# Moving a capacity comparison behind a weight split at the seam of two expert layers, and sharing a copy

## The chip, the cores and the metric

The kernel runs on one core of one Trainium2 chip. The metric is the time of one execution on the device in microseconds, from the core's own clock. A core has five engines that run their own instruction streams and meet through semaphores: TensorE (PE in the profile) for matrix products, VectorE (DVE), ScalarE (ACT), GpSimd (POOL) and SyncE (SP). DMAs are issued from the queues of SyncE, ScalarE and GpSimd. Before the change the kernel takes 393.19 us (median of three runs, 393.05 to 393.44).

## The reference

Three stages, each feeding the next, on N = 1536 tokens (2 batches of 768) with 512 features:

```
attention   state = gamma[h] * state + k_t v_t^T ;  y_t = scale * q_t state      (8 heads of 64)
layer 0     tokens with x @ w_skip > 0 choose the expert argmax(x @ w_gate) of 8
            out = x + gate * (relu(x @ w1[e]) @ w2[e])      w1 512x1024, w2 1024x512; other tokens pass
layer 1     every token chooses e = argmax(x @ w_gate) of 8
            the first `capacity` tokens of each expert, in token order, are kept
            out = gate * (relu(x @ w1[e]) @ w2[e]) for the kept ones, 0 for the others
```

The capacity in layer 1 is what the changed comparison is about: a token is kept only if fewer than `capacity` tokens ahead of it chose the same expert. Capacity is an input (384 here). The result is float32.

## The kernel before

**Stages.** The attention runs in chunks of 128 tokens and is over at about 75 us. Layer 0 follows, to about 195 us, then layer 1 to the end. In both layers experts are processed one after the other (a "job"): the rows of an expert's tokens are gathered by an indirect DMA of GpSimd into `xg`, turned on TensorE into `ps_t` (features on the partitions), copied to SBUF, multiplied by w1 in groups of 512 columns into `ps_h` (two banks by turns), passed through relu and multiplied by w2 into `ps_y`. The rows go back by an indirect store. A layer is a loop over "windows" of 128 (layer 0) or 256 (layer 1) tokens of each expert; one window does for the inputs here. Layer 0 takes 128 rows of each expert at a time, layer 1 takes 256.

**Precision.** Layer 1 (and the w2 products of layer 0) splits each fp32 operand in two parts that TensorE can take in its faster format: a high part (`w_hi`, `x_hi`, `h_hi`), which is a cast by ScalarE, and the rest (`w_lo`, `x_lo`, `h_lo`), which VectorE computes as original minus high part. A product is then three matmuls: w_hi x_hi, w_lo x_hi, w_hi x_lo. A job's weights come in four chunks of 1 MB (`raw`, loaded by SyncE, two jobs deep): 0 and 1 are w1, 2 and 3 are w2. Each has a split of 128x2048 elements on ScalarE (L732) and on VectorE (L1044). The matmuls of w1 are on L1425, those of w2 on L1453 and L1469. TensorE may start a chunk's matmuls when `hi_done` and `lo_done` of the chunk have come, and may write a bank of `ps_h` again when `h_hi` and `h_lo` of the group two before are made.

**Layer 1's choices while layer 0 ends.** The logits of layer 1 need the rows that layer 0 puts out. Those of the last two experts of layer 0 (the "late" rows, LATE = 2) come last, so their choices are made apart (`choose_late`, `rank_late`). The order of the tokens then has to be known over both kinds: `cross_counts` counts, with 24 small matmuls of the mask `above` with the late rows' choices `hot1`, how many late tokens stand ahead of each token and chose the same expert. `find_fits` (three small VectorE steps, L1149 to L1151) compares the sum of both counts with the capacity and writes `fits`. ScalarE stores `fits` to `flags` in HBM (L810), GpSimd gathers from it (L611), and VectorE uses it in layer 1's second job (L1125). `map_next` (L1342) is another set of small matmuls, which finds for each slot of an expert the token that goes there; its result in `ps_e` becomes the row numbers `slot_in` (L1167, L1169), with which GpSimd gathers the second job's rows (L539). The first job's rows are gathered earlier, by `gather_first` (L580). They come from `x_rows` as it stands then; the rows of the last expert of layer 0 that belong to them are added by matmuls of `late_hot` (L1566) into `ps_t`, on which `turn_first` (L1391) then accumulates the others.

**The order at the seam.** Each engine's queue is written out by hand, and it is strictly in order:

- TensorE, end of layer 0: L1566, then `above_ready`, `cross_counts` (which signals `crossed`), then `slots_ready` and the late map (signals `slots_mapped`). Layer 1: wait for `first_in` (the gather), `turn_first` (signals `first_half` after half of it and `turned` at its end), two filler matmuls on a zero tile (`keep_clock`, L1240), then `hidden(first, 0)`: it waits for `x_hi_done`, `hi_done[0]`, `lo_done[0]`. Its first 8 matmuls are w_hi x_hi, the next 8 w_lo x_hi, and before the third 8 it waits for `x_lo_done`.
- VectorE, end of layer 0: `choose_late(1)`, `rank_late(1)`, `late_hot`, `place` (L920), then a wait for `crossed` and `find_fits`. Layer 1: `split(first, 0)`, a wait for `slots_mapped`, L1167 and L1169, `split_x`, `split(first, 1)`, `relu` (h_lo, L1055) of group 0, `split(first, 2)`, and so on.
- ScalarE: the casts of chunks 0 and 1 of the first job, then `copy_first`, which copies both halves of `x_hi` (L745), the cast of chunk 2, h_hi of group 0 (L750), a wait for `fits_ready`, the store of the flags, the exponential, the cast of chunk 3.
- GpSimd: `gather_first` (L580, two DMAs), the stores of the last job of layer 0 (L564, L572), waits for stores and gathers to land, then in layer 1 the wait for the ids and the gathers of the second job.
- SyncE: the loads of the second job's weights wait for `first_in`.

`Chain` is a helper that lets each of a row of dependent VectorE steps signal a semaphore and wait for it; it counts its steps, and that count per window stands in the code (47 and 18). `hold` is a wait that also counts up a semaphore nobody reads.

## Time and profile before

| | us |
|---|---|
| median of the runs | 393.19 |
| the profiled execution | 393.83 |
| its span, first to last instruction | 392.0 |
| TensorE busy | 380.6 |
| VectorE busy | 260.8 |
| ScalarE busy | 171.6 |
| GpSimd busy | 83.8 |

The table's first line is of executions without the profiler, the others of the one execution that was profiled. The span lies inside the execution's time. "Busy" counts the time in which an engine works on an instruction; matmuls overlap in the pipeline, so TensorE's busy time is not time at its peak. The granted TensorE clock was full (1.00) over the span. The chain of work that ended last is followed back from the last instruction, at each step to what released it; what lies on it sets the end.

### The profile page before, as it was taken

What the parts mean: (1) busy time and instruction counts of PE and PEld (TensorE: products, weight loads), DVE (VectorE), ACT (ScalarE), POOL (GpSimd) and SP (SyncE); (2) the same over time, 40 slices, a digit from 0 to 9 for tenths busy, and PEclk for the clock granted to TensorE, in tenths of its full rate; (3) what the DMA queues carried; (4) which work ended last, traced back from release to release, by engine and by line L of the source; (5) the groups of instructions that cost most, each with busy time, mean ns of one, the idle gap of its engine ahead of it and who ended that gap; (6) DMA issues with size and microseconds to landing.
All of it is one profiled execution on the core that took longest, in us unless ns stands there. A gap on an engine that the chain in (4) does not pass through costs nothing.

```text
span 392.0 us, 7630 instructions
## 1 busy us (share of the span) xinstructions
PE 380.6 (97%) x2853; PEld 341.2 (87%) x2853; DVE 260.8 (67%) x468; ACT 171.6 (44%) x218; POOL 83.8 (21%) x83
## 2 busy tenths in 40 slices
PE   8999999999999999999889999999999999999996
PEld 5888887788899889988679898989989899898983
DVE  2876877759998889879396847364474636547340
ACT  2454453515324532451464256455454644445410
POOL 5110000240454142331432021402204030030103
PEclk9999999999999999999999999999999999999999
DMA  7999998389999999809599988666748557440102
GB/s 244 367 380 383 348 350 288 73 317 399 390 387 390 390 386 360 299 7 361 165 346 354 352 306 253 228 225 205 246 179 287 183 207 247 152 163 2 53 0 89
DMA packets 56018, 101.55 MB, mean 259 GB/s; under 512 B 6693, under 2 KB 18469, under 8 KB 55856
## 3 DMA queue, kind: packets, MB, share of 16 engines
q1 hardware_dynamic: 46048, 85.67, 61.7%
q0 software_dynamic: 4576, 11.71, 8.8%
q10 hardware_dynamic: 5360, 3.70, 3.1%
q8 instruction: 23, 0.38, 0.4%
q14 instruction: 11, 0.09, 0.1%
HBM read 89.91 MB, written 12.73 MB: 262 GB/s over the span
## 4 chain that ended last, share of the span: by engine, by line
PE 93%; DVE 2%; DMA 2%; issue 1%; ACT 1%; SPq 1%; POOL 0%; DVEq 0%; ACTq 0%; POOLq 0%
PE ps_h L1425 38%; PE ps_y L1453 31%; PE ps_r L1300 3%; PE ps_s L1253 3%; PE ps_o L1288 3%; PE ps_u L1267 3%; PE ps_y L1469 3%; PE ps_t L1383 2%; PE ps_o L1280 2%; DMA k_in<-in_k_rows 2%; PE ps_h L1240 1%; DVE w_lo L1044 1%; PE ps_t L1566 1%; PE ps_t L1492 1%; PE ps_e L1342 0%
## 5 line engine op out<-in xcount | busy, mean ns | idle before, releaser
L1044 DVE TENSOR_TENSOR w_lo<-raw,w_hi 128x2048 fp32r<-128x2048 f32 x48 | 109.1, 2288 | 19.8 <-ACT w_hi L732 18.2
L732 ACT CAST w_hi<-raw 128x2048 fp32r<-128x2048 f32 x48 | 90.7, 1909 | 4.0 <-PE ps_y L1453 2.9
L1055 DVE SCALAR_TENSOR_TENSOR h_lo<-ps_h,h_hi 128x512 fp32r<-128x512 f32 x48 | 33.1, 690 | 63.1 <-ACT h_hi L750 53.1
L750 ACT ACTIVATE h_hi<-ps_h 128x512 fp32r<-128x512 f32 x48 | 28.8, 599 | 96.9 <-PE ps_h L1425 93.9
L1453 PE MATMUL ps_y<-w_hi,h_hi 128*128 128x512 f32 x176 | 70.7, 402 | 0.0
L1453 PE MATMUL ps_y<-w_hi,h_lo 128*128 128x512 f32 x176 | 68.8, 391 | 0.0
L1453 PE MATMUL ps_y<-w_lo,h_hi 128*128 128x512 f32 x176 | 68.7, 390 | 0.0
L1425 PEld LDWEIGHTS ps_h<-x_f,raw 128*128 128x128 f32 x512 | 58.5, 192 | 1.3 <-issue 0.7
L1425 PE MATMUL ps_h<-x_f,raw 128*128 128x128 f32 x512 | 58.9, 275 | 0.3 <-issue 0.3
L1425 PE MATMUL ps_h<-x_hi,w_hi 128*128 128x256 f32 x256 | 41.1, 283 | 1.6 <-DVE w_lo L1044 1.6
L1425 PE MATMUL ps_h<-x_hi,w_lo 128*128 128x256 f32 x256 | 41.0, 283 | 0.0
L1425 PE MATMUL ps_h<-x_lo,w_hi 128*128 128x256 f32 x256 | 41.0, 283 | 0.0
L539 POOL DMA_INDIRECT xg<-x_rows,slot_in x14 | 15.3, 1096 | 114.4 <-ACT yo L761 106.6
L1453 PEld LDWEIGHTS ps_y<-w_hi,h_lo 128*128 128x128 f32 x176 | 33.0, 188 | 7.2
L1453 PEld LDWEIGHTS ps_y<-w_lo,h_hi 128*128 128x128 f32 x176 | 33.2, 188 | 5.9
L1453 PEld LDWEIGHTS ps_y<-w_hi,h_hi 128*128 128x128 f32 x176 | 33.1, 188 | 5.9
L1425 PEld LDWEIGHTS ps_h<-x_hi,w_hi 128*128 128x128 f32 x256 | 35.6, 191 | 2.5 <-issue 1.9
L1425 PEld LDWEIGHTS ps_h<-x_lo,w_hi 128*128 128x128 f32 x256 | 35.3, 192 | 0.0
L1425 PEld LDWEIGHTS ps_h<-x_hi,w_lo 128*128 128x128 f32 x256 | 35.2, 192 | 0.0
L539 POOL DMA_INDIRECT xg<-x_rows,slot_id x8 | 15.3, 1907 | 70.6 <-issue 47.5
L1077 DVE SCALAR_TENSOR_TENSOR product<-yo,w_wide 128x512 f32<-128x512 f32 x48 | 30.3, 689 | 0.0
L564 POOL DMA_INDIRECT out<-yo,slot_out x16 | 16.1, 1003 | 39.0 <-ACT yo L761 20.9
(175 smaller groups left out, 429.7 us busy)
## 6 DMA issues: line engine op xcount, KB each, us to landing
raw<-in_moe_w SPq DMA_DIRECT2D x64, 1024.0 KB
q_t<-in_q_cols SPq DMA_DIRECT2D x16, 192.0 KB, 6.1
k_t<-in_k_cols SPq DMA_DIRECT2D x16, 192.0 KB, 6.0
x_rows<-rows ACTq DMA_DIRECT2D x8, 384.0 KB, 5.4
k_in<-in_k_rows SPq DMA_DIRECT2D x15, 192.0 KB, 6.5
v_in<-in_v_rows SPq DMA_DIRECT2D x15, 192.0 KB, 6.4
out<-zero SPq DMA_DIRECT2D x1, 2816.0 KB
w_wide<-w_next SPq DMA_DIRECT2D x1, 2048.0 KB, 14.3
```

The lines of the kernel that those rows point to most:

```text
L539: nc.gpsimd.indirect_dma_start(out=job.rows_of(t), out_offset=None, in_=x, in_offset=bass.IndirectOffsetOnAxis(ap=ids[t], axis=0), bounds_ ...
L564: nc.gpsimd.indirect_dma_start(out=target, out_offset=bass.IndirectOffsetOnAxis(ap=rows_at, axis=0), in_=yo[:, job.par, t * DM:(t + 1) * D ...
L732: nc.scalar.copy(w_hi[c], raw[:, 4 * job.par + c, :]).then_inc(hi_done[c], 1)
L750: nc.scalar.activation(h_hi[:, g * 512:(g + 1) * 512], ps_h[:, g % 2, :], ACT.Relu).then_inc(h_hi_done[i], 1)
L1044: nc.vector.tensor_tensor(w_lo[c], raw[:, 4 * job.par + c, :], w_hi[c].bitcast(F32), ALU.subtract).then_inc(lo_done[c], 1)
L1055: nc.vector.scalar_tensor_tensor(out=h_lo[:, cols], in0=ps_h[:, g % 2, :], scalar=0.0, in1=h_hi[:, cols].bitcast(F32), op0=ALU.max, op1=AL ...
L1077: last = nc.vector.scalar_tensor_tensor(out=product[:, e], in0=yo[:, job.par, 0:DM], scalar=1.0, in1=w_wide[:, e], op0=ALU.mult, op1=ALU.m ...
L1253: last = pe.matmul(ps_s[:, p, a, c * P:(c + 1) * P], k_t[part, hp, toks], q_t[part, hp, toks], start=True, stop=True)
L1267: last = pe.matmul(ps_u[:, c * P:(c + 1) * P], k_dec[:, p, c].rearrange("p a d -> p (a d)"), v_in[:, hp, half * HC + c].rearrange("p a d - ...
L1288: last = pe.matmul(ps_o[a * D:(a + 1) * D, c * P:(c + 1) * P], v_in[:, hp, c0 + c, a, :], probs[:, p, a, c, :], start=False, stop=True, sk ...
L1425: last = pe.matmul(dst, wt[:, kk * QF + fb * P:kk * QF + (fb + 1) * P], xt[:, kk, :], start=(kk == 0 and z == 0 and not (first and g == 0 ...
L1453: last = pe.matmul(ps_y[:, t, :], ht, wt, start=(fb == 0 and z == 0), stop=(fb == 2 * QB - 1 and z == 2))
```

## The change

It does four things. The three steps of `find_fits` move in VectorE's queue from the end of layer 0 to layer 1's first job, behind `split_x` and ahead of `split(first, 1)`. The counts of `cross_counts` go to columns 128 to 223 of the bank `ps_e`, where the maps are at columns 0 to 31, instead of a bank of `ps_y`; TensorE does the late map ahead of them, and one semaphore, `slots_mapped`, tells of both (`crossed` goes). ScalarE copies only the first half of the first `x_hi`; VectorE copies the second in a new step `copy_half`, on whose semaphore `x_half_done` it waits itself before `split_x`. TensorE waits for `x_half_done` beside `x_hi_done`. ScalarE's wait for `fits_ready` becomes a plain one on this window's count.

```diff
--- before.py
+++ after.py
@@ -37,6 +37,7 @@
 LATE = 2
 GL = G + LATE
 PRE = 2 * P
+CROSS = P
 
 
 class Layer:
@@ -281,7 +282,7 @@
         first_in = sem("first_in")
         first_half = sem("first_half")
         late_placed = sem("late_placed")
-        crossed = sem("crossed")
+        x_half_done = sem("x_half_done")
         fits_ready = sem("fits_ready")
         flags_stored = sem("flags_stored")
         flags_in = sem("flags_in")
@@ -737,13 +738,8 @@
                     nc.scalar.copy(dst, ps_t[:, 0:KD * cap].rearrange("p (k n) -> p k n", k=KD)).then_inc(x_hi_done[i], 1)
 
                 def copy_first(job):
-                    for h in range(2):
-                        if h == 0:
-                            act.wait_ge(first_half, w + 1)
-                        else:
-                            act.wait_ge(turned[1], job.n + 1)
-                        last = nc.scalar.copy(x_hi[:, 2 * h:2 * h + 2], ps_t[:, h * 2 * cap:(h + 1) * 2 * cap].rearrange("p (k n) -> p k n", k=2))
-                    last.then_inc(x_hi_done[1], 1)
+                    act.wait_ge(first_half, w + 1)
+                    nc.scalar.copy(x_hi[:, 0:2], ps_t[:, 0:2 * cap].rearrange("p (k n) -> p k n", k=2)).then_inc(x_hi_done[1], 1)
 
                 def relu(job, g):
                     wait_hidden(act, layer, job, g)
@@ -806,7 +802,7 @@
                         copy_first(first)
                         split(first, 2)
                         relu(first, 0)
-                        hold(act, fits_ready, first_fits)
+                        act.wait_ge(fits_ready, w + 1)
                         act.dma_start(flags.rearrange("(p g) e -> p g e", g=G), fits[:, 0:G]).then_inc(flags_stored, 16)
                         nc.scalar.activation(ex[:], below[:], ACT.Exp).then_inc(exp_done[1], 1)
                         split(first, 3)
@@ -829,7 +825,6 @@
                         scale_y(last_two[1], by_block=True)
                 n_win = win.count()
                 base = n_win * (E // 2)
-                first_fits = n_win
 
 
         @block.vector
@@ -1048,6 +1043,11 @@
                     dve.wait_ge(x_hi_done[1], job.n + 1)
                     nc.vector.tensor_tensor(x_lo[:], ps_t[:, 0:KD * cap].rearrange("p (k n) -> p k n", k=KD),
                                             x_hi[:].bitcast(F32), ALU.subtract).then_inc(x_lo_done[1], 1)
+
+                def copy_half(job):
+                    dve.wait_ge(turned[1], job.n + 1)
+                    nc.vector.tensor_copy(x_hi[:, 2:4], ps_t[:, 2 * cap:4 * cap].rearrange("p (k n) -> p k n", k=2)).then_inc(x_half_done, 1)
+                    dve.wait_ge(x_half_done, w + 1)
 
                 def relu(job, g):
                     dve.wait_ge(h_hi_done[i], job.n * layer.groups + g + 1)
@@ -1145,14 +1145,14 @@
                     nc.vector.tensor_tensor(first_id[:], first_found[:], found[:, :, 1, 0], ALU.add).then_inc(first_ids, 1)
 
                 def find_fits(chain):
-                    counts = [at.rearrange("p (g e) -> p g e", e=E) for at in (ps_g[:, PRE:PRE + G * E], ps_y[:, 1, 0:G * E])]
+                    counts = [at.rearrange("p (g e) -> p g e", e=E) for at in (ps_g[:, PRE:PRE + G * E], ps_e[:, CROSS:CROSS + G * E])]
                     chain.step(nc.vector.tensor_scalar(tmp[:, 0:G], counts[0], cap_f[:, 0:1], None, ALU.subtract))
                     chain.step(nc.vector.tensor_tensor(tmp[:, 0:G], tmp[:, 0:G], counts[1], ALU.add))
                     nc.vector.tensor_scalar(fits[:, 0:G], tmp[:, 0:G], 0.0, None, ALU.is_lt).then_inc(fits_ready, 1)
 
                 win = Windows(dve, layer)
                 with dve.Fori(0, win.reg) as w:
-                    wchain = Chain(dve, win_link[i], w, (47, 18)[i])
+                    wchain = Chain(dve, win_link[i], w, (45, 20)[i])
                     hold(dve, window_stored[i], w + 1)
                     first = Job(layer, base, w, 0, 0)
                     if i == 1:
@@ -1191,7 +1191,9 @@
                             last = nc.vector.tensor_tensor(above[:, j], repeat(iota_b[:, 0:P], 1, G), repeat(offset[:, j], 2, P), ALU.is_gt)
                         last.then_inc(above_ready, 1)
                     else:
+                        copy_half(first)
                         split_x(first)
+                        find_fits(wchain)
                         split(first, 1)
                         relu(first, 0)
                         split(first, 2)
@@ -1219,8 +1221,6 @@
                         nc.vector.tensor_scalar(late_hot[:], iota_b[:], rank1[:, G + 1:G + 2], late_first[:, 0:1], ALU.is_equal, ALU.mult
                                                 ).then_inc(late_placed, 1)
                         place(1, [G + 1]).then_inc(slots_ready[1], 1)
-                        dve.wait_ge(crossed, w + 1)
-                        find_fits(wchain)
                     else:
                         wchain.step(nc.vector.tensor_scalar(rank1[:], rank1[:], -float(cap), None, ALU.add))
                         place(1, range(GL)).then_inc(slots_ready[1], 1)
@@ -1331,9 +1331,9 @@
 
                 for g in range(G):
                     for j in range(LATE):
-                        last = pe.matmul(ps_y[:, 1, g * E:(g + 1) * E], above[:, j, g, :], hot1[:, G + j, :],
+                        last = pe.matmul(ps_e[:, CROSS + g * E:CROSS + (g + 1) * E], above[:, j, g, :], hot1[:, G + j, :],
                                          start=g + j == 0, stop=j == LATE - 1, skip_group_check=True)
-                last.then_inc(crossed, 1)
+                return last
 
             def map_next(groups):
 
@@ -1398,6 +1398,8 @@
 
                     if c == 0 and part[0] == 0:
                         pe.wait_ge(x_hi_done[i], job.n + 1)
+                        if first:
+                            pe.wait_ge(x_half_done, w + 1)
                     if i == 0:
                         pe.wait_ge(raw_landed[4 * job.par + c], job.all_half * 16 + 16)
                     else:
@@ -1565,10 +1567,10 @@
                         for kk in range(KD):
                             pe.matmul(ps_t[:, kk * 2 * P:(kk + 1) * 2 * P], yo[:, 1, kk * P:(kk + 1) * P], late_hot[:],
                                       start=kk % 2 == 0, stop=False, skip_group_check=True)
+                        pe.wait_ge(slots_ready[1], w * 3 + 3)
+                        map_next([G + 1])
                         pe.wait_ge(above_ready, w + 1)
-                        cross_counts()
-                        pe.wait_ge(slots_ready[1], w * 3 + 3)
-                        map_next([G + 1]).then_inc(slots_mapped[1], 1)
+                        cross_counts().then_inc(slots_mapped[1], 1)
                     else:
                         output_by_block(last_two[1])
                         for kk in range(0, KD, 2):
```

## Rows read from the trace of the kernel before

**Rows 1.** The page: TensorE's busy time, share, instructions; shares of the chain by engine.

```profile
PE 380.6 (97%) x2853; PEld 341.2 (87%) x2853; DVE 260.8 (67%) x468; ACT 171.6 (44%) x218; POOL 83.8 (21%) x83
...
PE 93%; DVE 2%; DMA 2%; issue 1%; ACT 1%; SPq 1%; POOL 0%; DVEq 0%; ACTq 0%; POOLq 0%
```

**Rows 2.** The chain that ended last, around the seam: start us, us, what.

```profile
193.82 1.32 PE ps_y L1334 x24
...
195.16 0.33 DVE tmp L1149
...
195.51 0.27 DVE tmp L1150
...
195.80 0.05 DVE fits L1151
...
196.43 2.30 DVE w_lo L1044
198.73 0.14 issue
198.87 11.75 PE ps_h L1425 x96
```

**Rows 3.** Timeline of the seam: start, us, engine, line, operation, [idle before <-releaser].

```profile
189.26 3.70 ACT L732 CAST w_hi<-raw 128x2048 fp32r<-128x2048 f32 x2 [0.26 <-issue]
...
190.58 1.02 POOL L580 DMA_INDIRECT xg<-x_rows,first_id  x1 [0.30 <-issue]
...
191.69 0.28 DVE L920 TENSOR_SCALAR slots<-iota_b,rank 128x256 bf16<-128x256 bf16 x1
...
193.23 1.00 POOL L572 DMA_INDIRECT next_rows<-next_lg,slot_row  x1 [0.30 <-issue]
...
195.38 1.06 PE L1391 MATMUL ps_t<-iw,xg 128*128 128x128 f32 x8 [0.93 <-DMA xg<-x_rows,first_id]
195.40 2.19 SPq L439 DMA_DIRECT2D raw<-in_moe_w  x4
...
196.04 1.08 ACT L745 CAST x_hi<-ps_t 128x512 fp32r<-128x512 f32 x2 [3.08 <-PE ps_t L1391]
...
196.28 1.03 PE L1240 MATMUL ps_h<-zero 128*128 128x256 f32 x4
196.43 2.29 DVE L1044 TENSOR_TENSOR w_lo<-raw,w_hi 128x2048 fp32r<-128x2048 f32 x1 [0.42 <-issue]
...
198.64 0.17 DVE L1167 TENSOR_SCALAR found_id<-ps_e 128x16 f32<-128x16 f32 x1
...
198.93 1.22 DVE L1049 TENSOR_TENSOR x_lo<-ps_t,x_hi 128x1024 fp32r<-128x1024 f32 x1
...
199.89 1.04 POOL L539 DMA_INDIRECT xg<-x_rows,slot_in  x1 [5.66 <-DVE slot_in L1169]
...
200.06 2.28 DVE L1044 TENSOR_TENSOR w_lo<-raw,w_hi 128x2048 fp32r<-128x2048 f32 x1
...
200.86 1.12 PE L1425 MATMUL ps_h<-x_lo,w_hi 128*128 128x256 f32 x8
201.24 2.00 POOL L539 DMA_INDIRECT xg<-x_rows,slot_in  x1 [0.31 <-issue]
...
202.02 0.60 ACT L750 ACTIVATE h_hi<-ps_h 128x512 fp32r<-128x512 f32 x1 [3.10 <-PE ps_h L1425]
...
202.65 0.69 DVE L1055 SCALAR_TENSOR_TENSOR h_lo<-ps_h,h_hi 128x512 fp32r<-128x512 f32 x1 [0.30 <-ACT h_hi L750]
```

**Rows 4.** Busy us of each engine in two stretches behind the seam, clock, DMA.

```profile
199.00:212.00 13.00, 13.00 (x103) 12.74 (x104) 10.62 (x13) 4.62 (x7) 5.05 (x4) 1.00 1.01 369
212.00:386.00 174.00, 174.00 (x1162) 158.39 (x1161) 96.81 (x95) 83.77 (x78) 29.39 (x29) 1.00 0.58 196
```

**Rows 5.** The waits from 198 to 216: who waited for whom, us, times, longest.

```profile
POOL fits L611 <- DMA flags<-fits: 5.0, 1, 5.0
```

## The prediction

> **What bounds the kernel now.** I read the page first: TensorE is busy 97% of the span and holds 93% of the chain that ended last [rows 1]. So time can only come from a spot where the chain leaves TensorE. The chain in order of time [rows 2] shows such a spot at the seam of the two layers. TensorE ends its last small matmuls of layer 0 at 195.14. Then the chain runs on VectorE: three steps of the capacity comparison from 195.16, the loop's change of layer, and the split of the first weight chunk (w_lo) from 196.43 to 198.73. TensorE begins layer 1's first expert at 198.87. From there the chain is TensorE alone, and the windows say the same: busy 13.00 of 13.00 us and 174.00 of 174.00 up to 386 [rows 4]. What TensorE starts earlier at 198.87 the end gets back in full, unless a new gap opens behind it.
>
> The timeline of the seam [rows 3] tells what else stood ready at 198.87. The first expert's rows are turned from 195.38 (TensorE had waited for their gather, the last wait before it) to 196.44. ScalarE copied them to x_hi until 197.12. The weight's high part was cast long before: two chunks from 189.26 in 3.70, the first by about 191.1. VectorE had nothing from the end of its slots row (191.69 + 0.28 = 191.97) to 195.16. So w_lo ends last by 198.73 - 197.12 = 1.61 us, and only because it stands in VectorE's queue behind a comparison that waits for TensorE.
>
> **The change part by part.**
>
> 1. *The comparison leaves the end of layer 0.* VectorE goes on from 191.97. From the comparison's end (195.80 + 0.21 = 196.01) to w_lo there were 0.42 us of loop instructions [rows 3]; the same again puts w_lo at 192.4 to 194.7. It needs only the cast of 191.1. It is off the path by 2.5 us.
>
> 2. *TensorE's order.* The late map (2 matmuls) now runs ahead of the 24 cross counts, and one semaphore tells of both. The same 26 matmuls end at the same time, about 195.2. VectorE finds the ids at 195.2 to 195.6 (two of 0.17 and their gaps), where before they stood at 198.64. The bank of the counts costs nothing: the same instructions write elsewhere. Its price could only be a wait for an earlier reader of that bank, and that reader, VectorE's find_first, comes before the late rows in its own queue. I take 0, bounds 0 and 0.1.
>
> 3. *TensorE's turn of the rows* still waits for the gather: 195.38 to 196.44. This is the new start of the path. VectorE is idle by 195.6 and reaches the new copy's wait in time.
>
> 4. *The second half of x_hi on VectorE.* No row shows this copy. Nearest are VectorE's h_lo, which reads 512 elements of PSUM in 0.69, and x_lo, 1024 in 1.22 [rows 3]: 0.53 per 512 above 0.16 fixed. At one element a step the copy is 0.69; at two it would be 0.69 - 0.27 = 0.42, and that is the lower bound. The upper one is x_lo's 1.22. I take 0.69, that of the same size from the same memory, and start it at 196.50, so that it ends at 197.19. ScalarE's half ends at 196.04 + about 0.59 = 196.63 and no longer counts. The rows of ScalarE's two halves (1.08 together) say that moving the half saves nothing by itself: before, the second was done at 197.12.
>
> 5. *TensorE's start.* After the last semaphore there was 0.14 from w_lo's end to the first matmul [rows 2]. TensorE has one more semaphore to pass, in front of those of the weights; I put 0.03 on it, so 197.19 + 0.17 = 197.36. The clock fillers (from 196.28, 1.03, each issued 0.22 behind the last) leave room for a next matmul from about 197.15; they are the floor if the copy is the cheap one. Gain: 198.87 - 197.36 = **1.51 us**. With the copy at 0.42 TensorE starts near 197.2 (gain 1.65), with 1.22 at 197.9 (0.98).
>
> 6. *x_lo and what is behind.* x_lo now runs 197.22 to 198.44. TensorE asks for it after 16 matmuls (198.87 to 200.86 before, so 1.99): at 199.35. Cover 0.9. Then the comparison, 195.16 to 196.01 = 0.85 as before, from 198.4 to 199.2, then w_lo of chunk 1 from 199.15 to 201.43, against 200.06 before. VectorE's queue thus gains 0.9 where TensorE gains 1.5: the cover shrinks by 0.6. TensorE needs chunk 1 after 48 matmuls of 0.12 (96 in 11.75 [rows 2]), at 203.2, so 1.8 us remain. h_lo of group 0 is behind that split: 201.4 to 202.1, wanted at the same 203.2, 1.1 remain. Next split and h_lo of group 1: 202.0 to 205.0, wanted at 197.36 + 3 x 2.9 = 206.1, again 1.1. I cost the comparison in its new place at 0; if that cover were gone each us of it would count once.
>
> 7. *Who waits for the comparison.* ScalarE's store of the flags, after its h_hi of group 0. h_hi started at 202.02, now 200.5, and ends at 201.1; fits is there at 199.2. No wait. The flags' landing, for which GpSimd waited 5.0 us [rows 5], shifts 1.5 earlier with it, and its user comes in the next expert. Behind this wait in ScalarE's queue are the exponential and the cast of chunk 3, both unmoved relative to TensorE.
>
> 8. *GpSimd and the queues.* The ids are 3.2 us earlier, so the second expert's gathers (199.89 and 201.24 before) may go up to 3.2 earlier, or 0 if GpSimd is still held by its stores' landing. They are wanted after 96 + 24 matmuls, near 214.6: cover is over 10 us either way. SyncE's loads of the second expert's weights (issued from 195.40 on) hang on the same gather as before and don't move; ScalarE uses them from about 210, 14 us after. Cost 0.
>
> The w_lo of step 1 now lies over GpSimd's store from 193.23. The rows show what that does: the gather that began 0.17 ahead of a w_lo took 1.04, that begun inside it took 2.00, to 0.9 behind its end [rows 3]. So the store would end at 194.7 + 0.9 = 195.6 instead of 194.23. Nobody on the path waits for it. The Trainium skill, page "SBUF — State Buffer", section "Who interferes with whom", says that a VectorE instruction with two SBUF inputs contends with a GpSimd instruction that reads SBUF and not with one that only writes it, and infers that generating descriptors is therefore untouched by it. By that rule alone the first gather, issued before w_lo, is safe, and the trace's 2.00 against 1.04 would be GpSimd's read of the ids.
>
> The sum is 1.51. The profiled execution took 393.83 us, 1.83 around a span of 392.0; it becomes 392.3. The median of the runs shown is 0.64 lower, 393.19, and I take the same gain off it: **391.7 us**. The page "VectorE: DVE Perf Modes", section "Why PSUM operands drop a tier", of the Trainium skill gives an fp32 read from PSUM one element a cycle; its tier table beside it allows a copy up to twice that. By the second the copy would be the short one; both say less than the gap between the two is worth, 0.15 us.
>
> **Rivals.**
>
> *B, the gather lands late (16%).* Before, its landing had 1.6 us of slack under w_lo, so no time of the kernel shows how it scatters; now it counts one to one. It was issued by 190.58 + 1.02 and ended TensorE's wait at about 195.3, 3.7 us later. For: it shares the engines with GpSimd's next two stores. Against: the weight loads, the big traffic, wait for the same landing and cannot be in its way. The loss of 0.4 to 1.1 of the gain gives 392.1 to 392.8; about two thirds of it are still faster by over 0.2%. The copy at 1.22 lands here too (392.2).
>
> *C, the gain is given back (7%).* TensorE starts at 197.4 but stands at group 2 or 3, because VectorE's queue has the comparison in front. That takes 1.1 us over the sum of step 6, more than the comparison itself lasts, so it would need waits that no row shows. Then 393.2. That the change doesn't do what it says would be the same time: w_lo still behind something that waits for TensorE.
>
> *D, slower (5%).* The early w_lo, 192.4 to 194.7, lies in the 3.7 us between the gather's issue and its landing. If it holds that gather as it held the one inside w_lo, the landing comes w_lo's 2.29 later, at 197.6. Turning (1.06), the copy and the waits follow as in steps 3 to 5, and TensorE starts at 197.6 + 2.07 = 199.7, 0.8 later than before: 394.0. It decides from a landing later than 195.3 + 1.5 = 196.8. Against it: the record of the gather ended 0.8 us before w_lo starts, and an issue just ahead of a w_lo was not stretched.
>
> **How the numbers follow.** A, the forecast, 72%: gain 1.0 to 1.85, the upper end if the gather lands before TensorE is free (turning from 195.2) and the copy is cheap, so 391.3 to 392.2. What a measurement of this kernel can tell from no change is about 0.2%, 0.79 us, that is under 392.4. Faster: A and 10 of B's 16, 82%. Within: the rest of B and C, 13%. Slower: D, 5%. The range leaves C and D out, reaches 0.1 below A and takes all of B: 391.2 to 392.8.
>
> **What would show it.** In the profile after: w_lo before 195 and no VectorE wait on the cross counts in layer 0; a VectorE copy to x_hi of about 0.69 from 196.5; the first matmul of layer 1 at 197.4 with x_hi, not w_lo, as what ended its wait; the comparison behind x_lo; TensorE without gap from there to 385. It is wrong if the first matmul starts after 198, or if the windows behind it show TensorE below full.

## The result and the profile after

| us | before | after |
|---|---|---|
| median of the runs (four each) | 393.31 (393.05 to 394.22) | 390.82 (390.50 to 391.47) |
| the profiled execution | 393.83 | 391.47 |
| its span | 392.0 | 389.6 |
| TensorE busy | 380.6 | 380.2 |

The ratio is 0.9935, interval [0.9913, 0.9956]: 2.5 us faster, where 1.5 were forecast. 390.82 lies 0.4 below the range. The same pair is run on three chips (A, C and D) below, and the gain is not the same there. Two executions of these later runs lie far off and are in none of the ratios: 426.35 us of the kernel before on chip A and 962.53 us in compare_only.

The chain of waits after, around the seam (start us, us, what), which answers to [rows 2]:

```profile
189.73 4.72 DMA xg<-x_rows,first_id
194.45 0.14 issue
194.59 1.07 PE ps_t L1391 x8
195.66 0.87 PE ps_h L1240 x4
196.52 11.70 PE ps_h L1427 x96
```

VectorE is gone from it. The path is now the gather, TensorE's turn of the rows and layer 1's first group. The chain puts the fillers between the two, since TensorE was busy with them; the copies of `x_hi`, for which the first group waits, run beside them. The timeline of the same stretch answers to [rows 3]:

```profile
190.99 1.99 PE L1568 MATMUL ps_t<-late_hot,yo 128*128 128x256 f32 x8 [0.17 <-DVE late_hot L1221]
...
191.15 2.29 DVE L1039 TENSOR_TENSOR w_lo<-raw,w_hi 128x2048 fp32r<-128x2048 f32 x1
192.38 1.92 POOL L573 DMA_INDIRECT next_rows<-next_lg,slot_row  x1 [0.30 <-issue]
...
192.82 0.20 PE L1342 MATMUL ps_e<-carried,slots 128*128 128x16 bf16 x2
...
192.87 0.74 PE L1334 MATMUL ps_e<-hot,above 128*128 128x8 bf16 x24
193.77 0.17 DVE L1167 TENSOR_SCALAR found_id<-ps_e 128x16 f32<-128x16 f32 x1 [0.33 <-PE ps_e L1334]
...
194.59 1.07 PE L1391 MATMUL ps_t<-iw,xg 128*128 128x128 f32 x8 [0.98 <-DMA xg<-x_rows,first_id]
...
195.25 0.58 ACT L742 CAST x_hi<-ps_t 128x512 fp32r<-128x512 f32 x1 [3.13 <-PE ps_t L1391]
...
195.69 0.69 DVE L1049 CAST x_hi<-ps_t 128x512 fp32r<-128x512 f32 x1 [1.55 <-PE ps_t L1391]
...
196.42 1.22 DVE L1044 TENSOR_TENSOR x_lo<-ps_t,x_hi 128x1024 fp32r<-128x1024 f32 x1
...
196.44 1.22 PE L1427 MATMUL ps_h<-x_hi,w_hi 128*128 128x256 f32 x8
...
197.56 0.31 DVE L1149 TENSOR_SCALAR tmp<-ps_g,cap_f 128x96 f32<-128x96 f32 x1
...
198.19 0.21 DVE L1151 TENSOR_SCALAR fits<-tmp 128x96 f32<-128x96 f32 x1
198.32 2.28 DVE L1039 TENSOR_TENSOR w_lo<-raw,w_hi 128x2048 fp32r<-128x2048 f32 x1
198.99 2.50 POOL L540 DMA_INDIRECT xg<-x_rows,slot_in  x1 [0.31 <-issue]
```

The first split of layer 1 runs 191.15 to 193.44, while the gather is on its way. TensorE starts layer 1 0.06 after VectorE's copy has ended (195.69 + 0.69 = 196.38), and 0.79 after the turn (194.59 + 1.06). Before, that was 198.87 - 196.44 = 2.43 [rows 3]. The comparison is behind x_lo. Behind the seam nothing is lost (us and busy us of TensorE first; answers to [rows 4]):

```profile
212.00:386.00 174.00, 173.79 (x1156) 157.19 (x1154) 95.22 (x94) 81.31 (x78) 29.62 (x30) 1.00 0.56 194
```

TensorE's last matmul ends at 385.79, hence the missing 0.21. From layer 1's first matmul to the last of w2 there are 187.24 us, 187.18 before. In every trace of this study but one it is 187.18 to 187.24; in stream_shift it is 189.18, which is explained there.

**Where the time came from.** The two profiled executions don't yet differ in the changed code when they differ first. The first `ps_u` matmul of the attention, and the `late_hot` matmul at the seam, before:

```profile
8.00 0.94 PE L1267 MATMUL ps_u<-v_in,k_dec 128*128 128x128 f32 x6 [0.53 <-ACT k_dec L684]
191.82 1.99 PE L1566 MATMUL ps_t<-late_hot,yo 128*128 128x256 f32 x8 [0.17 <-DVE late_hot L1219]
```

and after:

```profile
7.05 0.83 PE L1267 MATMUL ps_u<-v_in,k_dec 128*128 128x128 f32 x6
```

with `late_hot` at 190.99. So 0.83 of the profiled 2.36 us lie ahead of the change; the first `ps_u` matmul is 0.95 earlier already. The rest is the seam. I count from the `late_hot` matmul to layer 1's first, and call it the seam time: 198.87 - 191.82 = 7.05 before, 196.44 - 190.99 = 5.45 after, a gain of 1.60, less 0.06 behind it.

### The profile page after: what moved, and what is told of

The parts are those of the page before. It is cut to its first block, busy times and chain, and to the rows that moved or that the text cites. A ratio compares the mean times of both kernels' runs of the same rounds, so it can differ in the third digit from the quotient of the medians.

```text
span 389.6 us, 7629 instructions
## 1 busy us (share of the span) xinstructions
PE 380.2 (98%) x2853; PEld 341.3 (88%) x2853; DVE 261.6 (67%) x469; ACT 170.8 (44%) x217; POOL 85.0 (22%) x83
## 4 chain that ended last, share of the span: by engine, by line
PE 92%; DMA 3%; issue 1%; SPq 1%; DVE 1%; ACT 1%; POOL 0%; ACTq 0%; POOLq 0%; DVEq 0%
PE ps_h L1427 38%; PE ps_y L1455 31%; PE ps_r L1300 3%; PE ps_o L1288 3%; PE ps_s L1253 3%; PE ps_y L1471 3%; PE ps_u L1267 3%; PE ps_t L1383 2%; PE ps_o L1280 2%; PE ps_h L1240 2%; DMA k_in<-in_k_rows 1%; DMA xg<-x_rows,first_id 1%; SPq L430 0%; SPq L418 0%; SPq L417 0%
```

## The experiments

All are edits of one of the two kernels. A to D are four chips; the changed kernel itself was not run on chip B. Each ratio is against runs of the kernel before on the same chip; "seam time" is from the one profiled execution of each. The gather's "landing" is the last of its pieces to arrive, and it is counted, like the seam time, from the `late_hot` matmul.

| kernel | median us | ratio [95%] | seam time | turn's end to first matmul |
|---|---|---|---|---|
| chip A: before_again | 393.84 | 0.9992 [0.9978, 1.0007] | 7.05 | 2.47 |
| after_again | 391.05 | 0.9922 [0.9903, 0.9941] | 5.66 | 0.79 |
| compare_only | 391.62 | 0.9935 [0.9912, 0.9957] | 5.26 | 0.73 |
| copy_only | 395.21 | 1.0038 [1.0016, 1.0060] | 7.88 | 3.14 |
| chip B: fill_gap | 392.64 | 0.9999 [0.9990, 1.0008] | 6.32 | 1.92 |
| wlo_late | 392.57 | 0.9991 [0.9981, 1.0000] | 6.04 | 1.32 |
| cross_behind_turn | 390.82 | 0.9955 [0.9942, 0.9969] | 4.74 | 0.83 |
| early_halves | 390.91 | 0.9950 [0.9935, 0.9965] | 5.07 | 0.24 |
| chip C: after_ref | 391.73 | 0.9975 [0.9967, 0.9984] | 5.66 | 0.79 |
| stream_shift | 393.51 | 1.0031 [1.0012, 1.0050] | 4.72 | 0.79 |
| shift_early | 393.12 | 1.0019 [1.0006, 1.0033] | 4.27 | 0.24 |
| before_shift | 395.11 | 1.0058 [1.0045, 1.0071] | 6.32 | 2.45 |
| chip D: before_third | 392.79 | 0.9997 [0.9988, 1.0006] | 6.32 | 1.81 |
| after_third | 391.60 | 0.9965 [0.9952, 0.9979] | 5.55 | 0.79 |
| shift_bf16 | 391.18 | 0.9957 [0.9944, 0.9969] | 4.71 | 0.79 |
| shift_bf16_early | 390.64 | 0.9952 [0.9934, 0.9969] | 4.46 | 0.24 |

### The pair again, and each half of the change alone (chip A)

before_again and after_again are the two kernels as they stand.

> The kernel before, unchanged, run as if it were a new one. Theory 1 (the 0.9 us of the profiled pair that lies ahead of the change, at the opening of the attention, is scatter between executions): this run's profile may open with its first ps_u matmul anywhere from 7.0 to 8.0 us, and the time is within 0.2% of the kernel before. Theory 2 (that 0.9 us belongs to the program, by its layout or its code): the first ps_u matmul is at 8.0 again, and the time is within 0.2% as well. The run alone tells the size of a difference that means nothing.

> The changed kernel, unchanged, on another chip and in more rounds. Theory 1 (opening is scatter, the change is worth the seam alone): 1.5 to 1.7 us faster than before, ratio 0.9957 to 0.9962; the first ps_u matmul anywhere from 7.0 to 8.0. Theory 2 (the opening belongs to the program): 2.4 to 2.6 us faster, ratio 0.9935 to 0.9939, with the first ps_u matmul near 7.05 again.

The opening changed sides. The first `ps_u` matmul of before_again:

```profile
6.98 0.83 PE L1267 MATMUL ps_u<-v_in,k_dec 128*128 128x128 f32 x6
```

against 7.98 in after_again. It belongs to neither program; the opening scatters by about 1 us. Nor does it carry to the seam in full: `late_hot` stands at 190.93 and 190.92 here. The seam gained 1.39 (7.05 to 5.66).

compare_only takes the comparison's move and TensorE's order, and leaves both halves of `x_hi` to ScalarE:

```diff
# against after
-                        copy_half(first)
                         split_x(first)
                         find_fits(wchain)
# and copy_first copies both halves again, TensorE waits for x_hi_done alone
```

> The changed kernel with both halves of the first x_hi copied by ScalarE, as before; the comparison, the bank and TensorE's order stay changed. Theory 1 (the whole gain at the seam is w_lo going ahead of the comparison; the shared copy is worth nothing): from the last matmul of the first turn (L1391) to the first w_hi x_hi matmul as in the changed kernel within 0.1 us, because ScalarE's second half ended 0.68 us after the turn before and VectorE's ends 0.73 after it now; time within 0.1 us of the changed kernel. Rival (the copy on the second engine is part of the gain): TensorE starts 0.3 to 0.6 us later than in the changed kernel and the time is that much longer.

```profile
194.92 1.06 PE L1395 MATMUL ps_t<-iw,xg 128*128 128x128 f32 x8 [0.85 <-DMA xg<-x_rows,first_id]
...
195.58 1.07 ACT L746 CAST x_hi<-ps_t 128x512 fp32r<-128x512 f32 x2 [2.99 <-PE ps_t L1395]
...
196.71 1.21 PE L1429 MATMUL ps_h<-x_hi,w_hi 128*128 128x256 f32 x8
```

ScalarE ends both halves at 196.65 = 0.67 after the turn; TensorE starts 0.73 after the turn, against 0.79 with the shared copy. At the seam the shared copy saves nothing: the comparison's move, with the split that it lets go ahead, is the whole gain there. The time doesn't settle it. compare_only was expected within 0.1 us of the changed kernel and its median is 0.57 above it (0.49 without the execution of 962.53), with intervals that overlap, although its profiled seam is 0.4 shorter (the gather landed at 3.34, in after_again at 3.68).

copy_only is the reverse: the shared copy in the kernel before.

```diff
# against before
                         dve: w_lo, found_id, slot_in
+                        copy_half(first)
                         split_x(first)
```

> The kernel before with only the second half of the first x_hi copied by VectorE, TensorE waiting for it; the comparison stays at the end of layer 0 and w_lo behind it. Theory 1: VectorE reaches the copy only behind w_lo and the ids, at 199.05 of the kernel before's time, ends it 0.69 later, and TensorE starts at 199.8 in place of 198.87: 0.9 us slower at the seam, ratio 1.0023. Rival (the shared copy is worth something by itself, by freeing ScalarE 0.4 us earlier): within 0.2 us of the kernel before.

```profile
195.84 2.29 DVE L1039 TENSOR_TENSOR w_lo<-raw,w_hi 128x2048 fp32r<-128x2048 f32 x1 [0.42 <-issue]
...
198.05 0.17 DVE L1167 TENSOR_SCALAR found_id<-ps_e 128x16 f32<-128x16 f32 x1
...
198.34 0.68 DVE L1049 CAST x_hi<-ps_t 128x512 fp32r<-128x512 f32 x1
...
199.08 1.22 PE L1428 MATMUL ps_h<-x_hi,w_hi 128*128 128x256 f32 x8 [2.27 <-DVE x_hi L1049]
```

The copy stands in VectorE's queue behind the split and the ids and costs 0.83 of seam time. The edit is harmful alone, and harmless only where the comparison and the split have left.

The granted clock is the other thing that chip A shows. Of 22 executions of the kernel before that the runs were compared with, 9 had a mean clock of 0.995 to 0.996 and took 394.08 to 395.24 us, some 1.4 more than the others; of before_again's own twelve it was 4. Of copy_only 8 of 12 had 0.991 to 0.996; of after_again and compare_only none. TensorE stands idle for 1.6 us just ahead of layer 1 in before_again, 2.3 in copy_only, and not at all in after_again and compare_only, where the fillers last until the copy is done. On chips B, C and D no execution of the two kernels shows such a clock; in before_third the idle time is 0.94, for a reason that follows. No kept trace of the kernel before or of copy_only has the lower clock in it, so it isn't shown where in the kernel it fell.

### Does the idle time cost clock? The split late, but the comparison gone; two more (chip B)

fill_gap puts three more filler units into the gap of the kernel before (10 matmuls on L1240 instead of 4):

```diff
-                    keep_clock(ps_h[:, 0, :], 1 + i)
+                    keep_clock(ps_h[:, 0, :], 1 + 4 * i)
```

> The kernel before with three more filler units (256 columns each) behind the first turn of layer 1, so that TensorE works through most of its wait for w_lo. Clock theory (of 22 executions of the kernel before on the last chip 9 had a mean granted clock of 0.995 to 0.996 and took 394.1 to 395.2 us, the others, at 0.999 or 1.0, 392.7 to 394.0: TensorE's idle 1.6 us at the seam lets the granted clock fall in part of the executions): TensorE starts layer 1 at the same time in the profile, no execution shows a mean clock under 0.999, and the median is 0.3 to 0.7 us under the kernel before. Rival (the clock falls elsewhere, or by itself): the share of executions at 0.996 stays, median within 0.2 us.

Ratio 0.9999, TensorE's idle time ahead of layer 1 is gone, and the clock never fell on this chip without it either. The test decides nothing on chip A's lower clock.

wlo_late keeps all of the change, except that the first split stands at layer 1's start, behind the ids:

```diff
# against after, VectorE
-                        split(first, 0)        # ahead of the late rows' ids
...
+                        split(first, 0)
                         copy_half(first)
```

> The changed kernel with the first w_lo behind the ids in VectorE's queue; the comparison stays behind x_lo. So w_lo is late again, without a comparison in front of it. Theory (w_lo ending last is the whole seam, and the idle TensorE the rest): w_lo starts right behind the ids, 3.8 us after the first late_hot matmul (L1568), the copy follows it, TensorE starts layer 1 at 6.8 to 6.9 us after that matmul, against 7.05 before and 5.45 to 5.66 in the changed kernel; executions at a clock of 0.996 come back (3 to 6 of 10) and the median is within 0.5 us of the kernel before. Rival (the comparison's removal from the end of layer 0 is a gain by itself): at least 0.8 us under the kernel before.

```profile
194.64 2.29 DVE L1039 TENSOR_TENSOR w_lo<-raw,w_hi 128x2048 fp32r<-128x2048 f32 x1
195.21 1.06 PE L1390 MATMUL ps_t<-iw,xg 128*128 128x128 f32 x8 [1.04 <-DMA xg<-x_rows,first_id]
...
196.85 0.68 DVE L1049 CAST x_hi<-ps_t 128x512 fp32r<-128x512 f32 x1
...
197.59 1.22 PE L1426 MATMUL ps_h<-x_hi,w_hi 128*128 128x256 f32 x8 [0.45 <-DVE x_hi L1049]
```

The comparison is off the path here too, and yet the ratio is 0.9991. The seam time is 6.04, not the 6.8 to 6.9 expected, because VectorE found the ids early (from 2.78 after `late_hot`); the kernel before has 6.32 on this chip (fill_gap). But this doesn't show that the 0.85 us of comparison are worth nothing, for wlo_late keeps the shared copy as well, and VectorE's half now stands behind the split, as in copy_only. The split ends at 5.38 after `late_hot` and the copy at 5.98. An estimate from these rows: with both halves on ScalarE, done 0.67 after the turn (4.72) as in compare_only, and 0.14 from the split's end to the first matmul [rows 2], TensorE would start at about 5.5, 0.8 ahead of 6.32. By this estimate the split late, with the comparison out of its way, gets much the same as the split under the gather where the semaphore is prompt (5.55 in after_third). What each is worth alone was not run.

cross_behind_turn puts the 24 cross counts behind TensorE's turn, in the place of the fillers (their bank is that of `ps_y` again, and VectorE waits for them apart):

```diff
                         map_next([G + 1])            # now signals slots_mapped
-                        pe.wait_ge(above_ready, w + 1)
-                        cross_counts().then_inc(slots_mapped[1], 1)
...
-                    keep_clock(ps_h[:, 0, :], 1 + i)
+                        pe.wait_ge(above_ready, w + 1)
+                        cross_counts().then_inc(w_turn, 1)
```

> The changed kernel with the 24 cross counts behind the first turn of layer 1, in place of the filler there, in the old bank ps_y and with their own semaphore. TensorE is then free 1.3 us earlier for the turn, which leaves the gather's landing alone to decide when it starts. If the landing is what the profiles show (3.35 to 3.7 us after the first late_hot matmul), the turn starts no earlier and the cross counts (1.3 us) in place of 0.86 us of filler make the start of layer 1 0.4 to 0.6 later: 0.4 to 0.6 us slower than the changed kernel. If in most executions the gather lands earlier than in the profiled ones (which would explain a gain of 2.5 us in the medians against 1.5 in the profiles at an equal clock), the earlier turn gives it back: within 0.2 us of the changed kernel, or faster.

```profile
190.96 2.00 PE L1573 MATMUL ps_t<-late_hot,yo 128*128 128x256 f32 x8 [0.17 <-DVE late_hot L1222]
...
193.81 1.07 PE L1392 MATMUL ps_t<-iw,xg 128*128 128x128 f32 x8 [0.82 <-DMA xg<-x_rows,first_id]
```

It was expected 0.4 to 0.6 us slower than the changed kernel; at 0.9955 it is not, as far as other chips' ratios can be compared. The turn begins 2.85 after `late_hot`, not 3.60. It still waits for the gather, so the gather itself landed earlier (2.71). What that has to do with the counts is in the DMA records: TensorE's instruction queue fetches 16 KB in one piece (0.96 us on one of the 16 DMA engines), and it does so 2.99 us after `late_hot` in after, 5.56 in this kernel. The last piece of the gather lands 0.49 behind the start of that fetch in after; over the twelve traces with the fetch beside it that is 0.48 to 0.53.

early_halves lets TensorE begin with the first half of `x_hi`, the products with the second half behind it, and takes one filler of the two out:

```diff
-                            order = [(fl, z) for z in range(len(terms)) for fl in part]
+                            order = [(fl, z, kks) for kks in (range(2), range(2, KD)) for z in range(2) for fl in part]
+                            order += [(fl, 2, range(KD)) for fl in part]
+                            # x_half_done is waited for ahead of the first (fl, 0, second half)
...
-                    keep_clock(ps_h[:, 0, :], 1 + i)
+                    keep_clock(ps_h[:, 0, :], 1)
```

> The changed kernel, with TensorE starting layer 1 on the first half of x_hi: the w_hi and w_lo products of features 0 to 255 (8 matmuls, 0.96 us) run ahead of those of 256 to 511, only these wait for VectorE's half, and one filler unit in place of two. Theory (the path behind the change is gather, turn, copy): TensorE starts 0.4 to 0.55 us earlier after the end of the turn (0.25 to 0.35 in place of 0.79), the rest follows without a gap, and the time is 0.4 to 0.5 us under the changed kernel. Rival (x_lo or VectorE's queue becomes the bound): TensorE waits at the first x_lo matmul and less than 0.2 us is left.

```profile
195.17 1.06 PE L1391 MATMUL ps_t<-iw,xg 128*128 128x128 f32 x8 [1.14 <-DMA xg<-x_rows,first_id]
...
196.47 0.74 PE L1428 MATMUL ps_h<-x_hi,w_hi 128*128 128x256 f32 x4
```

0.24 from the turn's end to the first matmul, 0.55 less than after. The changed kernel has no run on this chip, so what it is worth in time isn't shown here. Nor is it shown that it takes two engines: in compare_only ScalarE alone ends its second half 0.67 after the turn, VectorE's ends 0.72 after it in after, and the second half is wanted only 1.06 behind the first matmul (197.53). A semaphore on ScalarE's first half might do as well; that kernel was not run.

### Is it the fetch that holds the gather? (chip C)

Small matmuls added at layer 0's start shift TensorE's instruction stream, and so the place of the fetches, without an edit at the seam:

```diff
-                        keep_clock(ps_h[:, 0, :], 4)
+                        keep_clock(ps_h[:, 0, :], 1)
+                        small_fill(ps_h[:, 0, :], 28)     # bf16 matmuls of 8 columns
...
-                        keep_clock(ps_h[:, 0, :], 6)
+                        keep_clock(ps_h[:, 0, :], 1)
+                        small_fill(ps_h[:, 0, :], 36)
```

in after (stream_shift), in early_halves (shift_early) and in before (before_shift); after_ref is the kernel after.

> The changed kernel once more, as the reference on this chip for the three beside it. Theory: the gain over before is the seam's 1.4 to 1.6 us, plus whatever the executions without a full profile show more of it: 1.5 to 2.5 us. In the profile the last piece of the first gather lands 0.49 us after the start of the 16 KB instruction fetch that is in flight there, as in every profile so far but one.

> The changed kernel with TensorE's two filler stretches at the start of layer 0 made of 64 small matmuls (8 columns) and two units in place of ten units: the same idle time filled with some 96 instructions more, so that TensorE's stream of code reaches each 16 KB boundary earlier. Fetch theory (every such fetch runs on one DMA engine for 0.96 us; the one at 2.7 to 3.2 us after the first late_hot matmul holds back the last piece of the first gather, which lands 0.49 after its start, at 3.2 to 3.7, where all others are down by 1.9 to 2.7): the fetch goes away from there, the gather has landed by 2.8, the turn starts at 2.8 to 3.5, and the time is 0.2 to 0.8 us under the changed kernel. Rival (the last piece is late by itself): landing at 3.3 to 3.7 again, time within 0.15 us.

> Both stream_shift and early_halves (TensorE starts layer 1 on the first half of x_hi). If both theories hold the two gains add: start of layer 1 at 4.1 to 4.8 us after the first late_hot matmul against 5.45 to 5.66 in the changed kernel, 0.6 to 1.2 us under the changed kernel. If the time is that of stream_shift, what early_halves saves is given back further down.

> The kernel before with the fillers of stream_shift. Theory: the gather lands by 2.8 us too, but w_lo at 7.0 hides it, so the time is within 0.2 us of the kernel before. Rival (the fillers or the shift of the code act elsewhere in the kernel): a difference of over 0.3 us, which would then be part of stream_shift's as well.

stream_shift at the seam:

```profile
192.12 1.99 PE L1575 MATMUL ps_t<-late_hot,yo 128*128 128x256 f32 x8 [0.18 <-DVE late_hot L1221]
...
194.99 1.07 PE L1396 MATMUL ps_t<-iw,xg 128*128 128x128 f32 x8 [0.24 <-DMA xg<-x_rows,first_id]
```

The fetch is now 2.58 ahead of `late_hot`, and the turn starts 2.87 after it, against 3.81 in after_ref on the same chip. Nothing at the seam was edited. after_ref itself gained 1.0 us over the kernel before, less than the 1.5 to 2.5 expected. In before_shift the landing is early too (2.67) and the seam time stays 6.32, since w_lo sets the end there: the landing counts only in the kernel after. But all three kernels are slower than expected, and the windows of stream_shift show one reason (us and busy us of TensorE first, its granted clock third from the end):

```profile
74.00:78.00 4.00, 2.70 (x79) 2.37 (x77) 3.62 (x17) 3.13 (x2) 2.29 (x3) 1.00 0.25 72
78.00:82.00 4.00, 3.50 (x15) 2.87 (x16) 3.97 (x9) 0.59 (x1) 3.70 (x2) 0.57 0.74 226
```

The 8-column matmuls keep TensorE busy for 2.70 of 4 us, and the granted clock falls to 0.5 (1.2 GHz) from 78.23, for 3.41 us (6.83 in the other two). In stream_shift's trace it isn't all: later on TensorE waits for the gather of a later expert, which no trace of the unshifted kernels shows.

```profile
239.95 1.09 PE L1388 MATMUL ps_t<-iw,xg 128*128 128x128 f32 x8 [1.77 <-DMA xg<-x_rows,slot_in]
```

The twelve executions spread from 391.65 to 395.98 us at clocks of 0.989 to 0.996, so how much of the loss is clock and how much such waits stays open.

### The same shift with thicker matmuls, and the pair once more (chip D)

The fillers are 30 and 46 bf16 matmuls of 128 columns.

> The kernel before, unchanged, for its profile beside that of the next one on the same chip. Two values of the seam have been seen in kernels with the old order at the seam (first late_hot matmul to the first matmul of layer 1): 7.05 where the 24 cross counts and the late map took until 3.35 after that matmul, and 6.32 where they took until 2.6. Theory (the gain differs from chip to chip because this term does): where it is 7.05 the changed kernel gains 1.4 us or more at the same clock, where it is 6.32 it gains 0.7 to 0.9.

> The changed kernel, unchanged, beside the one above. Theory: first late_hot matmul to first matmul of layer 1 in 5.4 to 5.7 us, whichever the time of the cross counts is, because the gather's last piece (0.49 after the start of the instruction fetch) lands behind them; so the difference of the two seams, 1.4 to 1.6 or 0.7 to 0.9, is the difference of the median spans within 0.3 us. Rival (something else than the seam differs between the two kernels): the spans differ by 0.5 us or more beyond the seams.

> The changed kernel with the two filler stretches at the start of layer 0 made of 76 bf16 matmuls of 128 columns in place of ten fp32 units of 256 columns: about as long and as busy, and some 112 instructions more. Stream_shift had the fetch out of the way (landing at 2.7 in place of 3.2 to 3.7, start of layer 1 at 4.7 in place of 5.5 to 5.7) and lost more than that because its thin fillers let the granted clock fall from 78.2 to 81.6 us. Theory: the landing is at 2.7 again, the clock stays, and the time is 0.3 to 1.0 us under the changed kernel. Rival: the clock falls again, and it is slower than the changed kernel by 1 us or more.

> The same with TensorE starting layer 1 on the first half of x_hi. Theory: start of layer 1 at 4.2 to 4.4 us after the first late_hot matmul (4.27 in shift_early), 0.4 to 0.5 us under shift_bf16; the fastest kernel of all, at 1.0 to 1.5 us under the changed one. Rival: the start is early but the median is that of shift_bf16.

The same windows in shift_bf16:

```profile
74.00:78.00 4.00, 3.50 (x74) 3.33 (x75) 3.15 (x18) 3.70 (x2) 1.80 (x2) 1.00 0.13 24
78.00:82.00 4.00, 3.67 (x45) 3.24 (x43) 4.00 (x2) 0.58 (x1) 3.39 (x3) 1.00 0.69 171
```

The clock holds, and the seam time is 4.71 against 5.55 in after_third, as expected. Of that 0.84 the median shows 0.42; the intervals overlap, so the size in the time isn't settled. shift_bf16_early, with 4.46, has the lowest median of all, 390.64 (389.92 to 392.48), 2.2 below before on its chip. Against after_third's 391.60 and shift_bf16's 391.18 the intervals overlap as well.

before_third shows the other half of the story: the seam of the *unedited* kernel takes 6.32 here, not 7.05. VectorE's wait for the cross counts in before_third, then in before_again:

```profile
191.87 1.99 PE L1566 MATMUL ps_t<-late_hot,yo 128*128 128x256 f32 x8 [0.17 <-DVE late_hot L1219]
...
194.49 0.32 DVE L1149 TENSOR_SCALAR tmp<-ps_g,cap_f 128x96 f32<-128x96 f32 x1 [2.47 <-PE ps_y L1334]
```

```profile
190.93 1.99 PE L1566 MATMUL ps_t<-late_hot,yo 128*128 128x256 f32 x8 [0.17 <-DVE late_hot L1219]
...
194.27 0.32 DVE L1149 TENSOR_SCALAR tmp<-ps_g,cap_f 128x96 f32<-128x96 f32 x1 [3.20 <-PE ps_y L1334]
```

2.62 after `late_hot` in before_third, 3.34 in before_again. The matmuls' records don't differ: in both the last of the 26 starts 2.46 after `late_hot`. Only its semaphore comes 0.7 later, in the first trace of before and in all four of chip A, and neither in the first trace of after nor in the twelve of chips B to D. The kernel before has this wait on its path (w_lo is behind it); after has not, since the gather lands later than either.

## Why the prediction was right, and where it failed

- **Step 1, the comparison leaves and w_lo moves under the gather:** right. From the end of the slots row 0.42 was put for the loop; it was about 0.02 (190.85 + 0.28 to 191.15). compare_only shows that this step is the whole gain at the seam.
- **Step 2, TensorE's order at 0:** right that the order costs nothing; the last of the 26 matmuls starts 2.46 behind `late_hot` in both. Wrong in their end: "about 195.2" is read from the 1.32 us of [rows 2], which last until the semaphore came. By its record the last matmul starts at 194.28 in that trace. The late semaphore is not in every trace.
- **Step 3, the turn bound by the gather:** right in kind, 3.60 after `late_hot` against 3.56 put.
- **Step 4, the copy at 0.69:** exact. The Trainium skill, "VectorE: DVE Perf Modes", "Why PSUM operands drop a tier", has an fp32 read from PSUM at one element a cycle; the row of 0.69 us agrees, and the faster tier of its table was not seen.
- **Step 5:** 0.06 from the copy's end instead of 0.17. With the turn's end to first matmul at 0.79 against 2.43, the seam gained 1.60 for the 1.51 forecast. That moving the copy's half saves nothing by itself was said, and the rows of compare_only agree (0.73).
- **Steps 6 to 8:** right; the 96 matmuls behind the seam take 11.70, 11.75 before. The second expert's gathers go 2.2 us earlier (0 to 3.2 forecast). GpSimd's wait for the flags is 4.4 (5.0 in [rows 5]). GpSimd's store inside w_lo took 1.92 and ended 0.86 behind it (0.9 forecast), and the second gather inside the next split 2.50. No one on the path waited.
- **Rival D** is refuted: the gather issued just ahead of the early w_lo landed 3.47 after `late_hot`, 3.42 before. **Rival C** is refuted by the windows. **Rival B** didn't come in the first pair for the same reason, but its idea holds: the landing now counts one to one, and it scatters from 3.2 to 3.7 in kernels with the fetch beside it (after_third 3.57, before_third 3.32). The rival looked only at a landing later than before; without the fetch beside it the gather lands up to 1.0 earlier.

**The step that failed** is the upper bound in "How the numbers follow": "A, the forecast, 72%: gain 1.0 to 1.85, the upper end if the gather lands before TensorE is free (turning from 195.2)". It let the turn begin no earlier than 195.2, 3.4 after `late_hot`, because of the reading in step 2. Where the semaphore is prompt it comes at 2.6, and where the gather lands early the turn begins at 2.85 (cross_behind_turn) and 2.86 (shift_bf16). Then layer 1 starts at 4.71 (shift_bf16), with the copy still at 0.69; against the 7.05 of the trace before that is a gain of 2.34, above the 1.85 put as the most. That such a landing is what the unprofiled executions of the first comparison had isn't shown. Its profiled pair gained 1.60 at the seam, as forecast, and the other 0.9 of the 2.5 us stays open.

The forecast also took the difference of two programs for the difference at the seam, with all else fixed. Three other things vary by as much as its margin:

1. What lies ahead of the seam. `late_hot` came 0.83 earlier in after than in before, and at the same time in the next pair. Over the 13 traces with unchanged fillers in layer 0 it stands at 190.92 to 191.88, on the average at 191.36 with the old order at the seam (five) and 191.35 with the new (eight). It explains a wide spread between single executions, not the difference of medians.
2. The semaphore of the cross counts, late by 0.7 on chip A and in the first trace. It is in before's time and not in after's. Where it is late, the seam gain is 1.4 to 1.6, and the time gained is 2.8 on chip A and 2.5 in the first comparison (where the trace of before has it late and that of after prompt). Where it is prompt, the seam gain is 6.32 - 5.55 = 0.77, and the time gained is 1.3 on chip D (0.9965, where 0.7 to 0.9 was expected) and 1.0 on chip C (0.9975); both medians after, 391.60 and 391.73, are inside the range. The forecast was made from a trace with the late semaphore, so this term is in its 1.51 and can't explain why the gain was larger; it explains why it is smaller on C and D.
3. The granted clock of chip A: 13 of 34 executions of before take some 1.2 us more there, which is about 0.5 of before's mean and nothing of after's. That idle time at the seam causes it is argued from the counts (no idle time: none, 1.6 us: 13 of 34, 2.3 us: 8 of 12), not shown; fill_gap ran on a chip where there was nothing to mend. In the first comparison all four executions of after had a full clock (0.999 or more); of before's only the profiled one's, 1.00, is known.

**What stays open.** On chip A the executions at full clock have mean spans of 391.7 and 389.2, a difference of 2.5, where the profiled pair has 1.4 at the seam; about 1 us is not accounted for. On chip D it is 391.0 against 389.9, 1.1 for 0.77. Between the chips both kernels move, and in opposite ways: before is 0.6 to 0.8 longer on A than on B, C and D (391.0, 390.9 and 391.1), which is about the late semaphore, and after is 0.7 shorter on A than on C and D (389.95 and 389.9), for which no trace shows a reason, since its profiled seam is 5.66 there as well. An earlier landing of the gather in the executions whose trace isn't kept would do it (it lands up to 1.0 earlier without the fetch beside it), and the spans of after_third fall in two groups (389.3, 389.3, 389.5 and 390.1, 390.6, 390.6), but no trace of a fast one is there.

Nor is known why the semaphore is late. It may not be the chip alone: the traces of the first pair and of chip A have only 11 to 14 of the 32 records of the first gather's arriving pieces, those of chips B to D 31 or 32, so something else differs in these six.

## What to carry to other kernels

- In a queue that is strictly in order, look for the long step that needs nothing new and stands behind a short one that waits. Here 2.3 us of split stood behind 0.85 us of comparison and its wait for TensorE; with the split under the gather the seam took 1.4 to 1.6 us less where the wait was long and about 0.8 less where it was short. How much of that the comparison's going is worth with the split left late was not separated.
- Moving half of a copy to a second engine saved nothing by itself. Starting on the first half took 0.55 us off the stretch behind the turn; whether that needs the second engine was not tried.
- A forecast from one trace should carry the scatter of what it holds fixed: the part ahead of the edit, and each semaphore on the old path that is off the new one. An edit that takes a wait off the path also takes that wait's scatter off, and the gain then differs between chips by as much as the wait does. And the new path has a scatter of its own, here the gather's landing, which can go below the one value that the trace shows.

## What the runs showed of the hardware that was not expected

- A 16 KB fetch of TensorE's instructions at the same moment holds back an indirect gather. In after the fetch starts 2.99 after `late_hot` and the last piece lands at 3.47; in after_ref 3.19 and 3.68. Moved away (cross_behind_turn, stream_shift, shift_early, before_shift, shift_bf16) the last piece lands at 2.67 to 2.76; in shift_bf16_early at 3.02, so it isn't all of the scatter. Which fetch meets which transfer depends on how many instructions stand ahead, so an edit far from the seam moved the seam by 0.9 us.
- The wait for the same last small matmul ends 0.16 after the start of its record in the traces of three chips and about 0.9 after it on another; the two traces of the first pair have one of each.
- Matmuls of 8 columns let the granted clock fall to 0.5 for 3.4 to 6.8 us, those of 128 columns in the same place did not.
